# Three-stage attention and MLP kernel: row sums inverted through a spread tile and one transpose, weight ring of four places

## The reference

```python
scores = q @ k.T / 8;  kth = 32nd largest of each row
attn = exp(where(scores >= kth, scores, -1e9) - rowmax)
attn = attn / (attn.sum(-1) + 1e-9)
x = attn @ v                          # 4 x 8 heads, 576 x 576, head size 64 -> 2304 x 512
x = (sigmoid(x @ w_gate) * (x @ w_val)) @ w_out      # inner size 1536
out = relu(x @ w_in) ** 2 @ w_out2                    # inner size 2048
```

## Time and profile before

| | |
|---|---|
| median of 3 runs | 1322.89 us |
| the profiled execution | 1320.97 us, span 1319.2 us |
| PE busy | 1200.1 us (91%) |
| DVE, ACT, POOL busy | 845.2, 817.8, 690.8 us |
| chain that ended last | PE 64%, POOL 17%, ACT 10% |

### The profile page before, as it was taken

The page is one execution under the profiler, slowest core; times in us unless marked ns, Lnnn a source line. Parts: engine busy times, 40 slices in busy tenths (PEclk is TensorE's granted clock), DMA queues, the critical chain, the costliest instruction groups (busy, mean ns, idle before and its releaser), DMA issues.

```text
span 1319.2 us, 21176 instructions
## 1 busy us (share of the span) xinstructions
PE 1200.1 (91%) x7200; PEld 1037.4 (79%) x7200; DVE 845.2 (64%) x1680; ACT 817.8 (62%) x1792; POOL 690.8 (52%) x625
## 2 busy tenths in 40 slices
PE   4455689888899999999999999999999999999999
PEld 3344588877788888878888888888888888899998
DVE  6777768788976666778657768884766676011130
ACT  5677778778777766787666657766555575311130
POOL 5666478778775555776535527744352553122130
PEclk9666689998999999999999999999999999999999
DMA  3676146655465565555654555656454445566665
GB/s 125 229 249 220 57 157 218 204 196 187 166 246 197 210 221 190 193 195 194 225 177 158 175 191 192 204 178 208 163 184 161 173 144 168 168 215 218 220 211 169
DMA packets 78874, 249.37 MB, mean 189 GB/s; under 512 B 8752, under 2 KB 9776, under 8 KB 78768
## 3 DMA queue, kind: packets, MB, share of 16 engines
q1 hardware_dynamic: 78768, 248.02, 54.8%
HBM read 207.62 MB, written 40.37 MB: 188 GB/s over the span
## 4 chain that ended last, share of the span: by engine, by line
PE 64%; POOL 17%; ACT 10%; issue 6%; DMA 3%; DVE 0%; SPq 0%; POOLq 0%; ACTq 0%
PE ps L464 17%; PE ps L466 17%; PE ps L465 17%; POOL below L716 4%; PE ps L401 4%; PE ps L417 4%; POOL ring L711 4%; PE ps L389 4%; POOL klo L698 4%; DMA w_raw<-w_in 3%; POOL qkh L703 2%; ACT qkh L499 2%; POOL full_buf L760 1%; ACT probs L526 1%; ACT below L509 1%
## 5 line engine op out<-in xcount | busy, mean ns | idle before, releaser
L637 DVE MAX8 top<-work 128x8 f32<-128x576 f32 x432 | 312.1, 750 | 5.0
L464 PE MATMUL ps<-xy_hi,ring 128*128 128x512 f32 (+2 forms) x800 | 306.4, 383 | 9.1 <-POOL xy_lo L739 3.9
L716 POOL TENSOR_TENSOR below<-scores,below 128x576 f32<-128x576 f32 x144 | 206.1, 1431 | 205.9 <-ACT below L516 204.7
L466 PE MATMUL ps<-xy_hi,ring 128*128 128x512 f32 (+2 forms) x800 | 297.8, 372 | 0.0
L465 PE MATMUL ps<-xy_lo,ring 128*128 128x512 f32 (+2 forms) x800 | 297.6, 372 | 0.0
L464 PE MATMUL ps<-g_hi,ring 128*128 128x512 f32 (+2 forms) x560 | 213.1, 380 | 4.0 <-POOL g_lo L750 2.4
L639 DVE MATCH_REPLACE8 work<-top,work 128x576 f32<-128x576 f32 x288 | 213.9, 743 | 0.0
L466 PE MATMUL ps<-g_hi,ring 128*128 128x512 f32 (+2 forms) x560 | 207.9, 371 | 0.0
L465 PE MATMUL ps<-g_lo,ring 128*128 128x512 f32 (+2 forms) x560 | 207.6, 371 | 0.0
L464 PEld LDWEIGHTS ps<-xy_hi,ring 128*128 128x128 f32 x800 | 151.9, 190 | 36.9 <-issue 9.2
L466 PEld LDWEIGHTS ps<-xy_hi,ring 128*128 128x128 f32 x800 | 151.8, 190 | 22.3
(11 more groups left out here) (55 smaller groups left out, 2088.7 us busy)
## 6 DMA issues: line engine op xcount, KB each, us to landing
ring<-w_split SPq DMA_DIRECT2D x273, 512.0 KB, 3.4
w_split<-ring SPq DMA_DIRECT2D x68, 512.0 KB, 2.9
w_raw<-w_in SPq DMA_DIRECT2D x90, 256.0 KB, 3.6
vt<-v_in SPq DMA_DIRECT2D x32, 320.0 KB, 4.7
raw<-qk_in SPq DMA_DIRECT2D x16, 512.0 KB, 5.5
raw<-qk_in SPq DMA_DIRECT2D x16, 416.0 KB, 4.8
raw<-qk_in SPq DMA_DIRECT2D x8, 576.0 KB, 4.4
raw<-qk_in SPq DMA_DIRECT2D x8, 480.0 KB, 4.9
```

Of the source, the lines that this page charges most:

```text
L464: nc.tensor.matmul(dst, w_hi, hi[:, k, 0:WIDTH[c]], start=(k == 0), stop=False)
L466: mm = nc.tensor.matmul(dst, w_lo, hi[:, k, 0:WIDTH[c]], start=False, stop=(k == parts * KT - 1))
L637: nc.vector.max(out=best, in_=sc if step == 0 else wk).then_inc(sel_step[t % 2], 1)
L716: nc.gpsimd.tensor_tensor(out=below[:, t % 2, :], in0=scores[:, t % 4, :], in1=below[:, t % 2, :], op=ALU.subtract).then_inc(mask_done, 1)
```

## The change

- The ring has four places instead of five, and splitting runs three blocks ahead instead of four. The 4 KB in each partition that this frees hold among others a new tile `rinv_q` (two buffers of 128 columns).
- The addition of 1e-9 goes from ACT to POOL (`add_eps`, a TENSOR_SCALAR), at the head of the slot in which the unit is turned.
- A new step on POOL, `spread_inverse`, copies the inverse (two columns) over the 128 columns of `rinv_q`. It stands behind the evacuations from the slot before.
- `times_v` begins with a wait for this copy and one 128x128 transpose of `rinv_q` into the same PSUM region; the two matmuls against the identity are gone. The tail matmul stands last instead of first.
- On POOL, `normalise` stands ahead of `mask` instead of behind it.

```diff
-RING = 5
+RING = 4
-AHEAD = 4
+AHEAD = 3
@@ times_v(u)
                 pe.wait_ge(pt_copied, u + 1)
+                pe.wait_ge(inv_spread, u + 1)
+                nc.tensor.transpose(ps[:, RR, 0:P], rinv_q[:, u % 2, :, :].rearrange("p h c -> p (h c)"),
+                                    ident[:, :]).then_inc(inv_turned, 1)
                 if u == FIRST_UNIT[g]:
                     pe.wait_ge(v_loaded[g % 2], 16 * (g // 2 + 1))
-                nc.tensor.matmul(ps[:, RR, PV:PV + P], vt[:, g % 2, KFULL * DH:KFULL * DH + P],
-                                 pt[:, u % 2, P * KFULL:P * KFULL + P], start=True, stop=False)
...
-                pe.wait_ge(inv_done, u + 1)
-                for h in range(2):
-                    m = 0 if UNITS[u][4] else h
-                    mm = nc.tensor.matmul(ps[DH * h:DH * h + DH, RR, 0:P], rinv[:, u % 2, m:m + 1].to_broadcast([P, DH]),
-                                          ident[:, :], start=True, stop=True)
+                mm = nc.tensor.matmul(ps[:, RR, PV:PV + P], vt[:, g % 2, KFULL * DH:KFULL * DH + P],
+                                      pt[:, u % 2, P * KFULL:P * KFULL + P], start=False, stop=True)
                 mm.then_inc(pv_done, 1)
@@ exp(t), ACT
-                if t == END[u]:
-                    n = 1 if part == 2 else 2
-                    act.wait_ge(exp_done, t + 1)
-                    wait(act, inv_done, u - 1)
-                    nc.scalar.activation(rsum_eps[:, u % 2, 0:n], rsum[:, u % 2, 0:n], ACT.Copy,
-                                         bias=1e-9).then_inc(sum_done, 1)
@@ invert(u), DVE
-                wait(dve, pv_done, u - 1)
+                wait(dve, inv_spread, u - 1)
@@ POOL
+            def add_eps(u):
+                heads = 1 if UNITS[u][4] else 2
+                pool.wait_ge(exp_done, END[u] + 1)
+                wait(pool, inv_done, u - 1)
+                nc.gpsimd.tensor_scalar(rsum_eps[:, u % 2, 0:heads], rsum[:, u % 2, 0:heads], 1e-9, None,
+                                        ALU.add).then_inc(sum_done, 1)
+            def spread_inverse(u):
+                pool.wait_ge(inv_done, u + 1)
+                wait(pool, inv_turned, u - 1)
...
+                nc.gpsimd.tensor_copy(rinv_q[:, u % 2, :, :], src).then_inc(inv_spread, 1)
@@ POOL, each slot
+                if s - TURN in UNIT_AT:
+                    add_eps(UNIT_AT[s - TURN])
+                if s - NORM in UNIT_AT:
+                    normalise(UNIT_AT[s - NORM])
                 if 0 <= s - MASK < NT:
                     mask(s - MASK)
-                if s - NORM in UNIT_AT:
-                    normalise(UNIT_AT[s - NORM])
                 for c, p in X_AT.get(s, []):
                     split_x(c, p)
                 for c, n in blocks_of(SHARES[s - 1][2]) if s else []:
                     evac(c, n)
+                if s - TURN in UNIT_AT:
+                    spread_inverse(UNIT_AT[s - TURN])
```

More of the change, by code:

```diff
@@ L202, in attention_mlps @@
         rinv = sb("rinv", [P, 2, 2])
+        rinv_q = sb("rinv_q", [P, 2, 2, B64])
         pt = sb("pt", [P, 2, NBLK * P])
@@ L263, in attention_mlps @@
         inv_done = sem("inv_done")
+        inv_spread = sem("inv_spread")
+        inv_turned = sem("inv_turned")
         transposed = sem("transposed")
@@ L406, in times_v @@
                 pe.wait_ge(pt_copied, u + 1)
+                pe.wait_ge(inv_spread, u + 1)
+                nc.tensor.transpose(ps[:, RR, 0:P], rinv_q[:, u % 2, :, :].rearrange("p h c -> p (h c)"),
+                                    ident[:, :]).then_inc(inv_turned, 1)
                 if u == FIRST_UNIT[g]:
                     pe.wait_ge(v_loaded[g % 2], 16 * (g // 2 + 1))
-                nc.tensor.matmul(ps[:, RR, PV:PV + P], vt[:, g % 2, KFULL * DH:KFULL * DH + P],
-                                 pt[:, u % 2, P * KFULL:P * KFULL + P], start=True, stop=False)
                 for k in range(KFULL):
                     for h in range(2):
+                        d = slice(DH * h, DH * h + DH)
                         v_at = (KFULL * DH + P) * h + DH * k
                         p_at = P * ((KFULL + 1) * h + k)
-                        nc.tensor.matmul(ps[DH * h:DH * h + DH, RR, PV:PV + P], vt[:, g % 2, v_at:v_at + DH],
-                                         pt[:, u % 2, p_at:p_at + P], start=False, stop=(k == KFULL - 1))
-                pe.wait_ge(inv_done, u + 1)
-                for h in range(2):
-                    m = 0 if UNITS[u][4] else h
-                    mm = nc.tensor.matmul(ps[DH * h:DH * h + DH, RR, 0:P], rinv[:, u % 2, m:m + 1].to_broadcast([P, DH]),
-                                          ident[:, :], start=True, stop=True)
+                        nc.tensor.matmul(ps[d, RR, PV:PV + P], vt[:, g % 2, v_at:v_at + DH],
+                                         pt[:, u % 2, p_at:p_at + P], start=(k == 0), stop=False)
+                mm = nc.tensor.matmul(ps[:, RR, PV:PV + P], vt[:, g % 2, KFULL * DH:KFULL * DH + P],
+                                      pt[:, u % 2, P * KFULL:P * KFULL + P], start=False, stop=True)
                 mm.then_inc(pv_done, 1)
@@ L522, in exp @@
                 wait(act, transposed, u - 1)
+                wait(act, sum_done, u - 1)
                 for h in range(2) if part == 2 else [part]:
@@ L717, in mask @@
                                         op=ALU.subtract).then_inc(mask_done, 1)
+            def add_eps(u):
[7 more added lines that the diff above has]
+                wait(pool, inv_turned, u - 1)
+                if UNITS[u][4]:
+                    src = rinv[:, u % 2, 0:1].unsqueeze(2).to_broadcast([P, 2, B64])
+                else:
+                    src = rinv[:, u % 2, :].unsqueeze(2).to_broadcast([P, 2, B64])
+                nc.gpsimd.tensor_copy(rinv_q[:, u % 2, :, :], src).then_inc(inv_spread, 1)
             def normalise(u):
@@ L728, in normalise @@
                     return
+                pool.wait_ge(inv_spread, u + 1)
                 nc.gpsimd.tensor_tensor(out=xf[0:B64, p, col:col + B64], in0=rp[0:B64, u % 2, PV:PV + B64],
```

## The result

The changed kernel takes 1344.88 us in the median of four runs (1343.46 to 1346.72), the kernel before on the same chip 1323.17. The ratio is 1.0167, with a 95% interval from 1.0147 to 1.0186. The forecast was 1330, so the direction was right and the size was not: 22 us slower where 7 were forecast. The profiled execution took 1344.60 us.

What follows compares the result with a forecast made beforehand. PE was taken to set the pace after 400 us, with engines waiting for each other before. -6.6 + 9 + 5 + 2 - 2 = +7.4 us on 1320.97 gave 1328.4, forecast as 1330; range 1327 to 1340.

Steps and rivals of the forecast that it cites:

- PE's saving per unit: In times_v, one transpose replaces two matmuls: 0.13 us a unit over 51 units after 400 us, -6.6 us.
- Late copies after 400 us: PE waits for POOL's copy before the product at seven of 51 units: +9 us, ends 0 and 15.
- 9 + 2: +9 us for late copies after 400 us, and +2 us for three ring loads coming late in chunk 1.
- The stretching by DVE's two-input operations: POOL's copy held up to 0.67 us by the shared port pair at seven units after 400 us: 4.7 us more.
- To 163 us: Up to 163 us, earlier normalise and ACT's lost addition against a later mask: -2 us, ends -6 and +5.
- 163 to 400 us: ACT and POOL set the pace, so 31 us of late products don't add up: +5 us, ends -3 and +25.
- The ring, in the same step: From 163 to 400 us, four places make loads and splits late, mostly covered by PE's 3 us lead: +2.5 us.
- The rival "much slower": Four-place ring is what PE waits for in chunk 0, ring and split waits over 15 us: 1348 us, chance 0.16.
- `normalise` ahead of the mask: The move on POOL shortens ACT's waits: -3 us to 163 us, -2 us from 163 to 400 us.
- The signs that were named: times_v 1.4 to 1.45 us; copy waits some 25 us to 400 us, 5 to 12 after; chunk 0 ring waits 5 to 10.

Runs made afterwards that it cites:

- experiment 1: The changed kernel with five ring places and splitting four blocks ahead, as before the change: 1344.08 us, ratio 1.0164.
- experiment 5: The kernel before with the inverse's two matmuls, and their wait for it, at the front of the product, no POOL copy: 1340.35 us, ratio 1.0134.
- experiment 6: The changed kernel with five ring places and POOL's copy right behind the mask, wait still at the front: 1325.92 us, ratio 1.0022.
- experiment 7: The changed kernel with five ring places, ACT's copy of the product behind the enlarging, and normalise behind the mask on POOL: 1335.65 us, ratio 1.0101.
- experiment 2: The kernel before with four ring places and splitting three blocks ahead, nothing else: 1333.71 us, ratio 1.0082.
- experiment 9: Four versions without POOL's copy, 1317.59 to 1321.07 us; with a DVE copy and late transpose, normalise behind the mask took 1318.53 us, ahead of it 1321.07.
- experiment 4: The changed kernel with the transpose and its wait at the end of the product, and five ring places: 1320.68 us, ratio 0.9988.

## Why the prediction was right or wrong

**PE's saving per unit: right, a little too large.** 0.13 us was taken, 0.09 is measured (1.56 to 1.47). These are also the medians of the 51 units after 400 us, so the term is -4.6 us instead of -6.6. With the transpose at the end the saving is 0.13 to 0.14.

**Late copies after 400 us: right in kind, and in the sum partly by luck.** From the first block of chunk 1 to the end the kernel lost 5.6 us; with the saving of 4.6 that makes 10.2 of loss, where 9 + 2 were forecast. Units 40, 42, 59, 60 and 76 waited, 9.8 us in all, 1.6 of which PE waited before too, for the transposed probabilities. Of the units forecast, 33 and 61 did not wait, and unit 42 waited 2.75 us where 0.9 was forecast: the misses cancel. The stretching by DVE's two-input operations, which gave the upper end, did happen. Five of the 80 copies took 556 to 757 ns instead of 290 (median), each begun beside DVE's subtraction, like this one of unit 39:

```profile
557.82 1.10 DVE L670 TENSOR_TENSOR g_lo<-full_buf,g_hi 128x512 fp32r<-128x512 f32 x1
...
558.32 0.76 POOL L729 COPY rinv_q<-rinv 128x128 f32<-128x128 f32 x1
```

None of the four after 400 us was at a unit where PE waited, so there it cost nothing.

**To 163 us: not settled.** -2 was forecast, +1.2 measured in one trace, inside the range given. Kernels with small changes have their first block anywhere from 161.1 to 166.2 us, so neither sign is shown.

**163 to 400 us: this step failed.** +5 was forecast, 16.8 measured. The lateness was read rightly: 31 us summed over the units, and in experiment 1's kernel PE waits 32.4 us. What failed is the step that they don't add up because "PE runs ahead of them", by 3 us. That lead was read at the MLP blocks (3.1 us in the median), and the late instruction is not an MLP block. It is the product, and its own reader `copy_pv` stood only 1.3 us behind it, with the pace-setting chain queued behind that reader. Experiments 5, 6 and 7 bear this out in turn: an early wait for the inverse itself costs nothing in this stretch, an earlier copy gives back 9.6 of the 14.3 us that the early wait costs, and taking ACT's and POOL's readers off the front of the chain gives back 7.6. That the late copy costs the time is shown; how its cost divides between the reader's queue on ACT, `normalise` on POOL and the half clock is not.

**The ring, in the same step: right that it would cost little on top, for the wrong reason.** 2.5 us were given to it, because PE's lead would cover it. Alone it costs 11 us (experiment 2). In the changed kernel its removal gives nothing back, because the late copy already holds PE (experiment 1). The rival "much slower" came near the time, 1348, and even its sign was met: PE's waits for loads and splits there are 16 us, over the 15 I had named. Its cause is still wrong: with the ring put back, the kernel takes 1344.08. A wait's size does not show that its removal gives time back.

**`normalise` ahead of the mask: wrong sign.** -2 and -3 us were counted, because ACT waited for `xf` at a few slots. Those waits did shrink, from 14.9 to 7.5 us up to the first block of chunk 1. But the move costs 2.5 us in the whole (experiment 9), because the mask stands behind a `normalise` that waits for ACT. In the changed kernel too POOL waits for ACT's copy of the product 101.8 us in all, where it was 13.4.

**The half clock was not counted at all.** The windows view showed 0.73 and 0.96 in the two stretches with idle time, which was the hint.

**The signs that were named.** `times_v` takes 1.47 us, just above the 1.4 to 1.45. The transpose waited for the copy 39.3 us up to the first block of chunk 1, where some 25 were named, and 9.8 after it, inside 5 to 12. Waits for loads and splits in chunk 0 were 16 us, not 5 to 10.

## What to carry to other kernels

A late instruction costs by the distance to its own first reader and by what is queued behind that reader, not by the general lead of its engine. Two waits on one engine for the same stretch can cover each other: take each away alone, and both, before saying what either costs. A helper step that an engine needs at the front of its work must have nothing long ahead of it in its own queue. Needed only at the end of that work it costs far less: with the copy in the very same queue, the mixed stretch of experiment 4 is 2.7 us longer than before, where it was 17.

## What the runs showed of the hardware that was not expected

- A change between 128-column and 64-column matmuls costs 0.17 us of PE in experiment 5; two more for each of 51 units made most of its 17 us.
- Behind idle time of some microseconds the product ran at a granted clock of 0.50: 1.98 us for 16 passes instead of 1.09, at 7 of 17 units in experiment 1's kernel.
- Spreading two columns over 128 took 290 ns on GpSimd and 229 ns on VectorE (medians). Beside a two-input step of the other engine it lasted until some 0.1 us after that step: up to 757 ns on GpSimd (5 of 80), up to 1453 on VectorE (37 of 80).
- The reciprocal over 128 columns took 945 ns where that of two columns took 157.
